# Dynamic convolution and MLP on one core: spreads of the weights' bounds in bf16, and the first scale of w_in ahead of the lo of x

## The chip, the cores and the metric

The kernel runs on one core of one Trainium2 chip. The metric is device microseconds of one launch, the median of several runs. Engines are named as in the profile: PE is TensorE's matmuls and PEld its weight loads, DVE is VectorE, ACT is ScalarE, POOL is GpSimd, SP issues most of the DMAs.

## The reference

Softmax weights over 7 taps and 8 heads make a causal dynamic convolution of x (4 x 4096 positions, 192 channels), and its result goes through a two-layer MLP with a leaky ReLU. All is float32.

```python
w = weight_gen - np.max(weight_gen, axis=-1, keepdims=True)
w = np.exp(w)
w = w / (np.sum(w, axis=-1, keepdims=True) + 1e-09)
x_pad = np.concatenate([np.zeros((B, pad, D), dtype=np.float32), x], axis=1)
idx = np.arange(S)[:, None] + np.arange(K)[None, :]
x_unf = x_pad[:, idx, :].reshape(B, S, K, H, group)
out = np.einsum('bshk,bskhg->bshg', w, x_unf).reshape(B * S, D)
h = out @ w_in                      # 16384 x 192 @ 192 x 2048
g = np.maximum(0.01 * h, h)
return (g @ w_out).astype(np.float32)   # 2048 x 192
```

## The kernel before

Each of the 128 partitions holds 128 consecutive positions, and a tile is 4 positions of each partition, so 512 rows; there are 32 tiles. The engines are programmed by hand, one function each (`pool`, `sp`, `act`, `dve`, `pe`), with semaphores between them; nothing reorders an engine's list.

The float32 products of the MLP are made from fp16 pieces. A value is scaled by a power of two, its fp16 rounding is the "hi", the remainder in fp16 the "lo"; a product is hi·hi + lo·hi + hi·lo (and some lo·hi of the last rows). The weights are split once at the start, in pieces of 512 columns: w_in into `whA`/`wlA` (its first 128 rows) and `whD`/`wlD` (its last 64 rows, with lo rows), w_out into `wo`. Each tile's x (the convolution's result) is split into `xs`, hi by ACT (`hi_of_x`), lo by DVE (`lo_of_x`, two instructions for each of the 4 rows of a tile), and transposed into `xT`: by TensorE for tiles 0 and 1, by DMA from tile 2 on.

A group of hidden units is 4 blocks of 128; there are 4 groups to a tile, and group n of the whole run is `hidden...(n)` on PE into the 4 banks `h_ps`. ACT makes `gh` (fp16) and `g` (float32) of each block in `leaky`, DVE or POOL subtracts them into `gl`, and PE projects `gh` and `gl` with `wo` into the output banks. A block of the next group may enter an `h_ps` bank when ACT's `g` of the former one is done (`s_g`).

The power of two for the weights comes from a bound, the sum of absolute values over rows. ACT sums |w_in| into `w_sum[:, 0, 0:3]` in three instructions (`abs_w_in`, semaphore `s_w_abs`) and |w_out| into `w_sum[:, 1, 0:3]` (`abs_wo`, `s_wo_abs`). `spread_top(n)` on PE (line 1248) brings the 128 partitions' sums to all partitions: three products of a column of `w_sum`, broadcast to 128 columns, with the identity `ident`, into `out_ps`. DVE's `w_scales(n)` then takes the maximum (line 843) and makes the scale of it in three small instructions (lines 655, 659, 664). n is 0 for w_in and 1 for w_out.

The order in the opening is this. PE: 15 junk products, `sum0` (the first tile's convolution added up by identity products in float32, line 1237), `spread_top(0)`, the transposes of tile 0's hi (line 994), 4 junk products, `hidden_by_pe(0)` (hi products at line 1022, transposes of the rest, lines 1027 to 1036 and 1105, 1108), `spread_top(1)`, then `first_steps` with `hidden_early(1)` (line 1049) and the projections (lines 1131, 1141). DVE: the softmax of the first taps, the products of the first convolution, `scales0`, row 0 of `lo_of_x(0)`, `w_scales(0)`, the hi piece of w_in that PE needs first (`split_hi(("A", 0))`, line 730), rows 1 to 3 of `lo_of_x(0)` (lines 743, 745), then `first_tile` with the lo pieces (line 735), `out_scale0` (with `w_scales(1)`), and `group(0)` (line 883). ACT: sums of |x|, of |w_in|, `hi_of_x(0)`, sums of |w_out| between copies of the transposed rows, then `leaky`.

Of the kernel before, what the change touches and what calls it, by code (L numbers as in the profile page):

```python
# [9 lines left out]
BF16 = mybir.dt.bfloat16  # L10
# [3 lines left out]
P = 128  # L14
# [51 lines left out]
def dynconv_mlp(nc, x, weight_gen, w_in, w_out, out):  # L66
    B, S, D = x.shape
    _, _, H, K = weight_gen.shape
    FF = w_in.shape[1]
    G = D // H  # L70
# [4 lines left out]
    SUB = 4  # L75
# [13 lines left out]
    with ExitStack() as ctx:  # L89
        def sb(name, shape, dt=F32):  # L90
            return ctx.enter_context(nc.sbuf_tensor(name, shape, dt))
# [15 lines left out]
        ident = sb("ident", [P, P])  # L107
# [4 lines left out]
        w_sum = sb("w_sum", [P, 2, 4])  # L112
# [173 lines left out]
        def sum0_of(j):  # L286
            return sums0[j // 2][:, j % 2 * D:(j % 2 + 1) * D]
# [324 lines left out]
        def _(dve):  # L612
# [26 lines left out]
            def softmax0(half, n):  # L639

                if n == 2:
                    dve.wait_ge(s_exp0, half + 1)
                elif n > 0:
                    dve.wait_ge(s_softmax0[half], n)
                r = slice(half * SUB * H, (half + 1) * SUB * H)
                softmax_op(half_taps(half).rearrange("p (r k) -> p r k", k=K), tap_stat[:, 0, r], tap_stat[:, 1, r], n
                           ).then_inc(s_softmax0[half], 1)
# [77 lines left out]
            def split_hi(piece):  # L725
                raw, hi, _ = pieces[piece]
                if piece[0] == "D":
                    dve.wait_ge(s_rawD[1 + (piece[1] > 0)], DMA)
                dve.wait_ge(s_w_scale, scales_done(piece))
                nc.vector.tensor_scalar(hi, raw, scale_of(piece), None, ALU.mult).then_inc(s_w_hi_v, 1)  # L730
# [3 lines left out]
                wait_hi(dve, piece)  # L734
                nc.vector.scalar_tensor_tensor(lo, raw, scale_of(piece), hi, ALU.mult, ALU.subtract).then_inc(s_w_lo, 1)

            def lo_of_x(t, first=0, last=SUB):

                for j in range(first, last):
                    x_j = sum0_of(j) if t == 0 else conv[:, j, :]  # L740

                    dve.wait_ge(s_x_hi, j // 2 * 2 + 2 if t == 0 else SUB * t + j + 1)
                    nc.vector.scalar_tensor_tensor(xs[:, j, 2 * P:3 * P], x_j[:, 0:P], x_scale[:, j:j + 1],  # L743
                                                   xs[:, j, 0:P], ALU.mult, ALU.subtract).then_inc(s_x_lo, 1)
                    nc.vector.scalar_tensor_tensor(xs[:, j, D:2 * P], x_j[:, P:D], x_scale[:, j:j + 1],  # L745
                                                   xs[:, j, P:D], ALU.mult, ALU.subtract).then_inc(s_x_lo, 1)
# [33 lines left out]
            def next_rows(m):  # L780

                convolve(m + 1, N_CONV - 1)
                lo_of_x(m + 1)
# [57 lines left out]
            def w_scales(n):  # L841
                dve.wait_ge(s_w_spread, n + 1)
                nc.vector.tensor_reduce(w_all[:, n:n + 1], out_ps[:, 1, 2 * n * P:2 * (n + 1) * P], AX_X, ALU.max).then_inc(s_w_back, 1)
                dve.wait_ge(s_w_back, n + 1)
                exponent(w_all[:, n:n + 1]).then_inc(s_w_scale, 1)
                dve.wait_ge(s_w_scale, 3 * n + 1)
                unscale_of(w_unscale[:, n:n + 1], w_all[:, n:n + 1]).then_inc(s_w_scale, 1)
                dve.wait_ge(s_w_scale, 3 * n + 2)
                scale_of_unscale(w_scale[:, n:n + 1], w_unscale[:, n:n + 1]).then_inc(s_w_scale, 1)
# [45 lines left out]
            def first_tile():  # L895
# [25 lines left out]
                group(2, 2, GROUP)  # L921
                lo_pieces(11, 12)
                lo_of_x(1)
                take_transposed(1)
                dve.wait_ge(s_chunk[1], DMA * 2)
# [42 lines left out]
            scales0()  # L968
            for n in range(2, 4):
                softmax0(1, n)  # L970
            lo_of_x(0, 0, 1)
            w_scales(0)
            split_hi(("A", 0))
            lo_of_x(0, 1, SUB)
            first_tile()
            second_tile()
            third_tile()
# [13 lines left out]
        def _(pe):  # L991
# [240 lines left out]
            def sum0():  # L1232
                for k in range(K - 1):

                    pe.wait_ge(s_prod0, 1 if k == 0 else k + 2 if k < K - 2 else K + 2)
                    for half in range(2):
# [3 lines left out]
                        if k == K - 2:  # L1240
                            ins.then_inc(s_sum0, 1)

            def spread_top(n):

                parts = ((0, 0), (1, 1), (2, 1))
                for k, (col, to) in enumerate(parts):
                    pe.wait_ge(s_w_abs if n == 0 else s_wo_abs, col + 1)
                    ins = nc.tensor.matmul(out_ps[:, 1, (2 * n + to) * P:(2 * n + to + 1) * P],
                                           w_sum[:, n, col:col + 1].to_broadcast([P, P]), ident[:], start=k == 0,
                                           stop=k == len(parts) - 1, skip_group_check=True)  # L1250
                ins.then_inc(s_w_spread, 1)

# [2 lines left out]
            pe.wait_ge(s_ident, 3)  # L1255
            sum0()
            spread_top(0)
            transpose_hi(0)
            warm_up(WARM_UP[1])
            hidden_by_pe(0)  # L1260
            spread_top(1)
            first_steps()
            for n in range(BY_PE * NG, N_GROUPS):
# [24 lines left out]
```

## Time and profile before

| what | us |
|---|---|
| median of 3 runs | 1034.67 |
| the runs | 1031.80, 1034.67, 1035.04 |
| the profiled execution | 1031.82 |
| its span, first to last instruction | 1030.0 |
| PE busy | 1021.7 (99%) |
| DVE busy | 938.8 (91%) |
| ACT busy | 634.3 (62%) |
| POOL busy | 550.8 (53%) |

The profile is of one execution, 28966 instructions long. Of its 40 equal slices PE has 39 at nine tenths or more, and the granted clock of TensorE is nine tenths or more in all. A busy PE is a modelled figure: matmuls are pipelined, so the starts are to be read rather than the durations. The opening, in which the weights are split, ends at about 50 us; the loop over tiles 2 to 31 follows.

### The profile page before, as it was taken

The numbers are of one execution on the slowest core, as the hardware profiler recorded it, in microseconds if no ns is written. First come the engines' busy times: TensorE is split into PE (matmuls) and PEld (weight loads), VectorE is DVE, ScalarE is ACT, GpSimd is POOL, SyncE is SP. The second block draws the span as 40 slices with busy tenths as digits, with TensorE's granted clock in tenths as the row PEclk, the third lists the DMA queues.
The fourth block names the chain that finished last, engine by engine and source line by source line (L and its number), as shares of the span: only waits on it lengthen the run. The fifth ranks groups of instructions, "written<-read, shape, count | busy, mean of one in ns | idle before, by whom it ended". The sixth has DMA issues, their size and how long they took to land.

```text
span 1030.0 us, 28966 instructions
## 1 busy us (share of the span) xinstructions
PE 1021.7 (99%) x12751; PEld 614.2 (60%) x12751; DVE 938.8 (91%) x1199; ACT 634.3 (62%) x1352; POOL 550.8 (53%) x375
## 2 busy tenths in 40 slices
PE   9999999999999999999999999999999999999998
PEld 4666655556556556655655655655565565566566
DVE  7989999999999999999999999999999999998611
ACT  7866665665556656556656555665565665566564
POOL 0114665555556655655655665565665566556543
PEclk9999999999999999999999999999999999999999
DMA  9421203112031310213112021210413112111100
GB/s 268 109 62 32 98 19 98 35 42 88 4 97 35 97 35 22 77 34 98 36 37 77 19 97 35 88 41 4 98 35 97 35 31 69 34 35 36 34 17 17
DMA packets 68309, 59.84 MB, mean 58 GB/s; under 512 B 56348, under 2 KB 60700, under 8 KB 66200
## 3 DMA queue, kind: packets, MB, share of 16 engines
q1 hardware_dynamic: 67196, 55.35, 18.2%
q0 software_dynamic: 864, 2.36, 1.3%
q8 instruction: 100, 1.64, 0.7%
q10 hardware_dynamic: 124, 0.29, 0.1%
q14 instruction: 25, 0.20, 0.1%
HBM read 29.34 MB, written 12.58 MB: 41 GB/s over the span
## 4 chain that ended last, share of the span: by engine, by line
PE 91%; DVE 6%; DMA 1%; ACT 1%; issue 0%; SPq 0%; POOL 0%; DVEq 0%; ACTq 0%; POOLq 0%
PE h_ps L1067 43%; PE out_ps L1177 22%; PE t_ps L1177 22%; PE out_ps L1131 1%; DVE prod L681 1%; PE h_ps L1049 1%; DVE gl L883 1%; DVE conv L697 1%; DMA rawD<-in_moe_w_in_dram 1%; PE out_ps L1141 1%; DMA prod<-prod 0%; DVE xs L743 0%; DVE xs L745 0%; ACT w_abs L559 0%; DVE gl L755 0%
## 5 line engine op out<-in xcount | busy, mean ns | idle before, releaser
L349 POOL TENSOR_TENSOR gl<-g,gh 128x512 f16<-128x512 f32 x360 | 543.5, 1536 | 411.1 <-ACT g L483 411.1
L481 ACT ACTIVATE gh<-h_ps 128x512 f16<-128x512 f32 x512 | 319.0, 623 | 370.8 <-PE h_ps L1067 361.0
L1177 PE MATMUL t_ps<-wo,gh 64*128 64x384 f16 (+1 forms) x1984 | 386.6, 317 | 0.9 <-ACT gh L481 0.9
L1177 PE MATMUL out_ps<-wo,gh 64*128 64x384 f16 (+1 forms) x1984 | 386.6, 317 | 0.0
L1067 PE MATMUL h_ps<-xT,whA 64*128 64x512 f16 x1920 | 364.3, 376 | 0.0
L483 ACT ACTIVATE g<-h_ps 128x512 f32<-128x512 f32 x512 | 323.4, 632 | 0.0
L681 DVE TENSOR_TENSOR prod<-xbuf,taps 128x768 f32<-128x768 f32 x186 | 273.3, 1485 | 0.0
L697 DVE TENSOR_TENSOR conv<-conv,prod 128x768 f32<-128x768 f32 x174 | 266.5, 1532 | 1.0
L1177 PE MATMUL t_ps<-wo,gl 64*128 64x192 f16 x1920 | 233.2, 243 | 1.4 <-DVE gl L755 1.4
L1177 PE MATMUL out_ps<-wo,gl 64*128 64x192 f16 x1920 | 233.2, 243 | 0.0
L1177 PEld LDWEIGHTS t_ps<-wo,gh 64*128 64x128 f16 x1984 | 181.3, 94 | 57.6 <-ACT gh L481 1.4
L1177 PEld LDWEIGHTS out_ps<-wo,gh 64*128 64x128 f16 x1984 | 181.3, 94 | 33.5
L1177 PEld LDWEIGHTS t_ps<-wo,gl 64*128 64x128 f16 x1920 | 169.0, 94 | 30.8 <-DVE gl L755 1.8
L1177 PEld LDWEIGHTS out_ps<-wo,gl 64*128 64x128 f16 x1920 | 169.0, 94 | 29.6
L1067 PE MATMUL h_ps<-xT,whD 64*128 64x512 f16 x960 | 182.2, 376 | 0.0
L1067 PE MATMUL h_ps<-xT,wlA 64*128 64x512 f16 x960 | 182.1, 376 | 0.0
L755 DVE TENSOR_TENSOR gl<-g,gh 128x512 f16<-128x512 f32 x120 | 108.6, 905 | 64.5 <-ACT g L483 62.9
L1067 PEld LDWEIGHTS h_ps<-xT,whA 64*128 64x128 f16 x1920 | 93.6, 94 | 99.7 <-issue 0.3
L1067 PE MATMUL h_ps<-xT,wlD 64*128 64x512 f16 x240 | 90.2, 376 | 0.0
L1067 PE MATMUL h_ps<-xT_again,wlD 64*128 64x512 f16 x240 | 90.2, 376 | 0.0
L1067 PEld LDWEIGHTS h_ps<-xT,whD 64*128 64x128 f16 x960 | 46.8, 94 | 56.8
L1067 PEld LDWEIGHTS h_ps<-xT,wlA 64*128 64x128 f16 x960 | 46.8, 94 | 42.6
(117 smaller groups left out, 715.0 us busy)
## 6 DMA issues: line engine op xcount, KB each, us to landing
xbuf<-in_x_dram SPq DMA_DIRECT2D x15, 1344.0 KB, 6.0
out_dram<-stage SPq DMA_DIRECT2D x31, 384.0 KB, 2.3
taps<-in_weight_gen_dram SPq DMA_DIRECT2D x16, 224.0 KB, 6.0
xT_again<-xT SPq DMA_DIRECT2D x29, 64.0 KB, 2.1
rawO<-in_moe_w_out_dram SPq DMA_DIRECT2D x4, 384.0 KB, 10.4
prod<-prod POOLq DMA_DIRECT2D x4, 384.0 KB, 4.3
rawA<-in_moe_w_in_dram SPq DMA_DIRECT2D x2, 512.0 KB, 8.0
xbuf<-in_x_dram SPq DMA_DIRECT2D x2, 384.0 KB, 7.0
```

What stands on the lines that cost most here:

```text
L349: nc.gpsimd.tensor_tensor(gl[:, q % RING, :], g[:, q % RING, :], gh[:, q % RING, :], ALU.subtract).then_inc(s_gl_p, 1)
L481: nc.scalar.activation(gh[:, q % RING, :], h_ps[q % GROUP][:], ACT.Prelu, alpha=SLOPE, scale=SHRINK0 if n < 2 * NG else SHRINK).then_inc(s ...
L483: nc.scalar.activation(g[:, q % RING, :], h_ps[q % GROUP][:], ACT.Prelu, alpha=SLOPE, scale=SHRINK0 if n < 2 * NG else SHRINK).then_inc(s_ ...
L681: ins = nc.vector.tensor_tensor(dst.rearrange("p (r g) -> p r g", g=G), rows, w.to_broadcast([P, SUB * H, G]), ALU.mult)
L697: ins = nc.vector.tensor_tensor(acc, acc, prod[:, k % PRODS, :], ALU.add)
L755: nc.vector.tensor_tensor(gl[:, q % RING, :], g[:, q % RING, :], gh[:, q % RING, :], ALU.subtract).then_inc(s_gl_v, 1)
L883: nc.vector.tensor_tensor(gl[:, at, :], g[:, at, :], gh[:, at, :], ALU.subtract).then_inc(s_gl_v, last - first)
L1049: nc.tensor.matmul(dst, w[:, c], xT_block(m % 2, b), start=w is whA and b == 0, stop=False)
L1067: ins = nc.tensor.matmul(h_ps[f % GROUP][:], w[rows, c], moved, start=first and half == f % 2, stop=last)
L1131: nc.tensor.matmul(out_of(m, j), gh[:, (m * NF + f) % RING, j * P:(j + 1) * P], wo[:, f, part, :], start=f == 0 and j % 2 == 0 and part == ...
L1141: ins = nc.tensor.matmul(out_of(m, j), gl[:, (m * NF + f) % RING, j * P:(j + 1) * P], wo[:, f, 0, :], start=False, stop=f == NF - 1, skip_ ...
L1177: ins = nc.tensor.matmul(dst, a[rows, (m * NF + f) % RING, j * P:(j + 1) * P], moved, start=i == 0 and k < 2 and a is gh and f == 0 and pa ...
```

## The change

Two things are changed. In `spread_top` both operands, a column of `w_sum` and the identity, are float32 tiles; now each is viewed as bf16 and every second element is taken, the upper 16 bits of each float32 (a cut without rounding; of 0 and 1 exact). The products are then bf16 products. Both spreads go through the function. On DVE, row 0 of `lo_of_x(0)` no longer stands ahead of `w_scales(0)` and the first hi piece, and the four rows follow in one call.

```diff
@@ DVE
-            def lo_of_x(t, first=0, last=SUB):
+            def lo_of_x(t):
-                for j in range(first, last):
+                for j in range(SUB):
@@ DVE, opening
             for n in range(2, 4):
                 softmax0(1, n)
-            lo_of_x(0, 0, 1)
             w_scales(0)
             split_hi(("A", 0))
-            lo_of_x(0, 1, SUB)
+            lo_of_x(0)
             first_tile()
@@ PE
+            def upper(a):
+
+                return a.bitcast(BF16).rearrange("p (n half) -> p n half", half=2)[:, :, 1]
+
             def spread_top(n):
@@
-                                           w_sum[:, n, col:col + 1].to_broadcast([P, P]), ident[:], start=k == 0,
+                                           upper(w_sum[:, n, :])[:, col:col + 1].to_broadcast([P, P]),
+                                           upper(ident[:]), start=k == 0,
                                            stop=k == len(parts) - 1, skip_group_check=True)
```

On DVE, behind the softmax of the second half of the first taps, before (xs is the split x, w_all the maximum, whA the hi piece):

```order
L625 TENSOR_SCALAR tap_stat<-tap_stat 128x32 [waits s_softmax01]
L743 SCALAR_TENSOR_TENSOR xs<-out_ps,x_scale,xs 128x128 [waits s_x_hi]
L745 SCALAR_TENSOR_TENSOR xs<-out_ps,x_scale,xs 128x64
L843 TENSOR_REDUCE w_all<-out_ps 128x1 [waits s_w_spread]
L655 TENSOR_SCALAR w_all<-w_all 128x1 [waits s_w_back]
L659 TENSOR_SCALAR w_unscale<-w_all 128x1 [waits s_w_scale]
L664 TENSOR_SCALAR w_scale<-w_unscale 128x1 [waits s_w_scale]
L730 TENSOR_SCALAR whA<-rawA,w_scale 128x512 [waits s_w_scale]
L743 SCALAR_TENSOR_TENSOR xs<-out_ps,x_scale,xs 128x128 [waits s_x_hi]
L745 SCALAR_TENSOR_TENSOR xs<-out_ps,x_scale,xs 128x64
```

and after:

```order
L625 TENSOR_SCALAR tap_stat<-tap_stat 128x32 [waits s_softmax01]
L843 TENSOR_REDUCE w_all<-out_ps 128x1 [waits s_w_spread]
L655 TENSOR_SCALAR w_all<-w_all 128x1 [waits s_w_back]
L659 TENSOR_SCALAR w_unscale<-w_all 128x1 [waits s_w_scale]
L664 TENSOR_SCALAR w_scale<-w_unscale 128x1 [waits s_w_scale]
L730 TENSOR_SCALAR whA<-rawA,w_scale 128x512 [waits s_w_scale]
L743 SCALAR_TENSOR_TENSOR xs<-out_ps,x_scale,xs 128x128 [waits s_x_hi]
L745 SCALAR_TENSOR_TENSOR xs<-out_ps,x_scale,xs 128x64
L743 SCALAR_TENSOR_TENSOR xs<-out_ps,x_scale,xs 128x128 [waits s_x_hi]
L745 SCALAR_TENSOR_TENSOR xs<-out_ps,x_scale,xs 128x64
```

The pair of row 0 moved from ahead of the maximum to behind the hi piece; five instructions passed it.

On PE, from the end of the first convolution's sum to the hi products of tile 0, before (a row with x3 or x4 is that many alike):

```order
L1237 MATMUL t_ps<-prod,ident 128x384
L1248 MATMUL out_ps<-ident,w_sum 128x128 [waits s_w_abs] x3
L994 MATMUL t_ps<-ident,xs 128x128 [waits s_x_hi]
L994 MATMUL t_ps<-ident,xs 128x128 x3
L1230 MATMUL h_ps<-junk 128x512 x4
L1022 MATMUL h_ps<-xT,whA 128x512 [waits s_w_hi_v,s_xT_a]
```

and after:

```order
L1236 MATMUL t_ps<-prod,ident 128x384
L1251 MATMUL out_ps<-ident,w_sum 128x128 [waits s_w_abs] x3
L993 MATMUL t_ps<-ident,xs 128x128 [waits s_x_hi]
L993 MATMUL t_ps<-ident,xs 128x128 x3
L1229 MATMUL h_ps<-junk 128x512 x4
L1021 MATMUL h_ps<-xT,whA 128x512 [waits s_w_hi_v,s_xT_a]
```

Nothing moved on PE; only the type in which the three products read their operands is another, and line numbers shift (1248 is now 1251, the lines between 743 and 1248 are one lower).

## Rows read from the trace of the kernel before

**Rows 1.** Busy us (instructions) of PE, PEld, DVE, ACT, POOL by stretch; then clock, DMA.

```profile
32.00:39.50 7.50, 7.18 (x58) 4.42 (x56) 7.50 (x10) 7.41 (x19) 2.72 (x3) 1.00 0.65 119
39.50:49.60 10.10, 10.04 (x88) 6.92 (x88) 9.84 (x14) 7.63 (x21) 0.00 (x0) 1.00 0.50 146
...
500.00:1000.00 500.00, 500.00 (x6408) 296.54 (x6406) 455.91 (x570) 304.65 (x649) 288.83 (x192) 1.00 0.17 48
```

**Rows 2.** Chain of waits, 15 to 24.5 us: start, us, what.

```profile
15.25 0.63 ACT xs L468 x2
...
18.32 0.26 DVE xs L743
18.57 0.19 DVE xs L745
...
19.02 0.20 DVE xs L745
```

**Rows 3.** Timeline of PE: start, us, group, [idle before <-releaser].

```profile
15.18 0.83 PE L1248 MATMUL out_ps<-ident,w_sum 128*128 128x128 f32 x6
16.55 0.40 PE L994 MATMUL t_ps<-ident,xs 128*128 128x128 f16 x4 [0.54 <-ACT xs L468]
...
18.01 1.02 PE L1022 MATMUL h_ps<-xT,whA 128*128 128x512 f16 x4 [0.21 <-DVE whA L730]
19.27 0.62 PE L994 MATMUL t_ps<-ident,xs 128*128 128x128 f16 x8 [0.24 <-DVE xs L745]
...
23.38 0.93 PE L1248 MATMUL out_ps<-ident,w_sum 128*128 128x128 f32 x6
24.15 0.38 PE L1049 MATMUL h_ps<-xT,whA 128*128 128x512 f16 x1
...
39.49 0.38 PE L1049 MATMUL h_ps<-xT,whA 128*128 128x512 f16 x1 [0.29 <-DVE wlD L735]
...
49.64 2.81 PE L1131 MATMUL out_ps<-wo,gh 128*128 128x192 f16 x32
```

**Rows 4.** Groups by line and shape, 13 to 25 us: busy us, mean ns, idle before.

```profile
L1248 PEld LDWEIGHTS out_ps<-ident,w_sum 128*128 128x128 f32 x12 | 1.6, 190 | 0.5 <-issue 0.2
...
L994 PE MATMUL t_ps<-ident,xs 128*128 128x128 f16 x12 | 1.0, 221 | 0.8 <-ACT xs L468 0.5 <-DVE xs L745 0.2
...
L994 PEld LDWEIGHTS t_ps<-ident,xs 128*128 128x128 f16 x12 | 0.7, 98 | 1.5 <-DVE xs L745 0.7 <-ACT xs L468 0.7
```

**Rows 5.** Timeline of ACT in the opening.

```profile
15.06 0.18 ACT L559 ACTIVATION_READ_ACCUMULATOR w_abs<-rawA 128x1 f32 x1
...
17.19 0.59 ACT L472 COPY xT<-t_ps 128x512 f16<-128x512 f16 x1
...
19.01 0.22 ACT L453 ACTIVATION_READ_ACCUMULATOR wo_abs<-rawO 128x1 f32 x1
...
25.74 0.65 ACT L483 ACTIVATE g<-h_ps 128x512 f32<-128x512 f32 x1
```

**Rows 6.** Timeline of DVE in the opening.

```profile
15.90 0.35 DVE L743 SCALAR_TENSOR_TENSOR xs<-out_ps,x_scale,xs 128x128 f16<-128x128 f32 x1 [1.00 <-ACT xs L468]
...
16.36 0.41 DVE L843 TENSOR_REDUCE w_all<-out_ps 128x1 f32<-128x256 f32 x1
...
17.38 0.49 DVE L730 TENSOR_SCALAR whA<-rawA,w_scale 128x512 f16<-128x512 f32 x1
...
24.35 0.42 DVE L843 TENSOR_REDUCE w_all<-out_ps 128x1 f32<-128x256 f32 x1 [0.42 <-PE out_ps L1248]
```

**Rows 7.** The loop: DVE's gl by line, one meeting with POOL, its stretch.

```profile
L755 DVE TENSOR_TENSOR gl<-g,gh x120: 677/680/1643, 93.5 to 1022.0; 128x512 f16<-128x512 f32 x120
...
229.18 4.70 POOL L349 TENSOR_TENSOR gl<-g,gh 128x512 f16<-128x512 f32 x3 [4.37 <-ACT g L483]
229.40 1.64 DVE L755 TENSOR_TENSOR gl<-g,gh 128x512 f16<-128x512 f32 x1
...
231.10 0.25 PE L1177 MATMUL t_ps<-wo,gl 64*128 64x192 f16 x1 [1.35 <-DVE gl L755]
...
220.00:250.00 30.00, 28.65 (x378) 17.28 (x376) 28.36 (x35) 16.77 (x35) 16.77 (x12) 1.00 0.26 84
```

**Rows 8.** Groups of PE, 1 to 7.3 us: the junk products at the start.

```profile
L1230 PE MATMUL h_ps<-junk 128*128 128x512 f16 x15 | 6.4, 616 | 1.2 <-DVE junk L948 1.2
```

## The prediction, made before the changed kernel ran

> **What bounds the kernel now.** I read the page first, then the busy time by stretch, then the engines' timelines of the opening, because all of the change lies before 25 us. TensorE has 99% of the span, and is busy for 500.00 of 500.00 us between 500 and 1000 us [rows 1]. So the time is the start of TensorE's dense work plus its length. The change takes nothing out of the loop over the tiles. It can only move the moment at which the loop is entered, and by no more than the slowest path to it moves.
>
> Two engines share the lead in the opening. Up to 24 us it passes between them: the chain goes from ScalarE's xs rows at 15.25 to VectorE, which holds it up to 19.22 (row 0 of lo of x, the scale of w_in, the first hi piece, rows 1 to 3), then to TensorE, and at 24.35 VectorE has waited 0.42 us for TensorE's second spread [rows 2, 6]. From there to 49.6 VectorE is nearly full (7.50 of 7.50 us, 9.84 of 10.10), and TensorE too [rows 1]. Where the two meet, TensorE starts right behind VectorE's pieces: hidden group 3 at 39.49 behind a wlD piece, and at 49.64 the products of the last w_out piece, whose lo VectorE makes just before [rows 3]. So what counts at the end is how much earlier VectorE's queue runs after its second maximum, with TensorE's own saving as the second bound.
>
> **The change, part by part.**
>
> *Spread 0 in bf16.* Before, three float32 products run as six matmuls from 15.18 to 15.18 + 0.83 = 16.01 [rows 3]. As bf16 there should be three like the transposes of x (128x128, 16 bits): a weight load of 98 ns and a product of 221 ns in the mean, and eight of them in 0.62 us, which with some 0.22 for the last leaves (0.62 - 0.22) / 7 = 0.057 us from start to start [rows 3, 4]. The third of them waits for ScalarE's last sum of |w_in|, there at 15.06 + 0.18 = 15.24 [rows 5]. With 0.04 us for a signal and 0.24 from load to end the spread is in PSUM at 15.52. VectorE, idle until 15.90 now, can start its maximum at about 15.60, one more signal and a rounding up. Bounds: not before 15.50 (the bare load and product), and not after 16.05 (as float32, and a signal). Plain 16-bit rows are the nearest to it, but none of them skips every second element, which is why I keep the float32 end.
>
> The Trainium skill, page "FP8 and Floating Point Precision", section "TensorE Precision Notes", has true float32 as four passes through the array; by it the products of a spread would shrink to a quarter, and the six matmuls for three products in the row agree with more than one pass. Its page "TensorE: Matmul & The Clock Gate", section "Back-to-back issue gap", speaks for less gain: about 81 ns a product of 128 columns in a stream of loads and products. By it three would take 0.24 us instead of the 0.17 used below, and the sum would stay, since VectorE is the later one there.
>
> *The scale and the first hi piece ahead of lo of x.* Before, VectorE idles 1.00 us for the xs rows, does row 0 at 15.90, and starts the maximum at 16.36 [rows 6]. After, the maximum starts at 15.60, **0.76 us** earlier. The scale follows, and the hi piece ends at 17.38 + 0.49 - 0.76 = 17.11 instead of 17.87. TensorE gets little from that directly: its hi products at 18.01 need also ScalarE's copy of the transposed rows, which ends at 17.19 + 0.59 = 17.78 and doesn't move [rows 3, 5]. That is 0.09 us, and hidden again, for the next thing on TensorE is the transposes at 19.27, and these wait for the last row of lo of x.
>
> Row 0 now stands behind the scale, and a row costs 0.26 + 0.19 = 0.45 us [rows 2]. The eight lo instructions end at 19.22 - 0.76 + 0.45 = 18.91: **0.31 us** earlier (bounds: 0.41 earlier, 0.14 later). TensorE's four hi products, started at 17.92, free it at 17.92 + 4 x 0.215 = 18.78, before that. From here all shifts by 0.31: the transposes to 18.96, the copies of them (ScalarE is free for them at 19.01 + 0.22 = 19.23), the lo piece of w_in, hidden group 0, and ScalarE's leaky activations [rows 3, 5].
>
> *Spread 1 in bf16.* Before, TensorE spends 23.38 to 24.15 on it, 0.77 us, and VectorE is ready at 24.35 - 0.42 = 23.93 [rows 3, 6]. After, three products occupy 3 x 0.057 = 0.17 us, so TensorE saves 0.60. The spread starts at 23.38 - 0.31 = 23.07 and is in PSUM by 23.07 + 0.11 + 0.24 = 23.42. VectorE's queue reaches it at 23.93 - 0.31 = 23.62, so VectorE itself is late now, and the maximum comes at 23.62: 24.35 - 23.62 = **0.73 us** earlier. Whether a product takes 0.06 or 0.11 us doesn't matter.
>
> *TensorE behind it.* It could enter hidden group 1 at 23.24 instead of 24.15, 0.91 us earlier. But the fourth block of the group needs the PSUM bank that ScalarE's fourth g frees; that g ends at 25.74 + 0.65 = 26.39 and moves by 0.31 only, to 26.08 [rows 5]. Each block is four products of 0.215 us, so the fourth starts at 24.15 + 3 x 0.86 = 26.73 before, and at 26.12 after: 0.61 us earlier. TensorE keeps that until it meets VectorE's pieces, which are 0.73 earlier. By 39.49, where it idled 0.29 us for wlD, it has 0.61 + 0.29 = 0.90 to spare and takes all of VectorE's 0.73 [rows 3]. The same at 49.64. What VectorE reads in between (ScalarE's hi pieces and g) was there earlier than it was asked for, since VectorE never idles; the DMA additions for tile 1 are started by its products and so move with it. Behind 49.64 TensorE is full, and the 0.73 stays.
>
> **Sum.** -0.76 + 0.45 = -0.31 at 19 us; a further -0.42, the idle time that goes at 24.35; together **-0.73 us**. Bounds: -0.83 (both spreads at their best) and +0.14 (bf16 no quicker, so that only the loss of the swap is left). The profiled execution took 1031.82 us with a span of 1030.0, so by it the sum is 1031.09. It lies at the low end of the runs of before (1031.80, 1034.67, 1035.04), which stand in two groups some 3 us apart. Against the median it is 1034.67 - 0.73 = 1033.94. A measurement here tells about 0.3%, 3.1 us, from no change, so the whole gain is under it.
>
> **The rivals.**
>
> *The same sum, but the median falls in the lower group.* Two of four executions of before lie near 1031.8. How such groups can come about: VectorE's gl takes 680 ns in the median and up to 1643 where GpSimd works on gl at the same time, and TensorE stalled 1.35 us behind one such here [rows 7]; a few more or fewer make 3 us. (The Trainium skill, "GPSIMD Engine Reference", section "1. Specifications", says that GpSimd shares its SBUF interfaces with VectorE instructions of two SBUF inputs; the trace agrees, 1643 against 677 ns.) Time: 1031.80 - 0.73 = 1031.07, 0.35% under the median of before.
>
> *Nothing gained, or a part.* If upper halves are read no faster than float32, all is 0.14 later: 1034.8. If ScalarE's 0.31 decides somewhere behind 24 us: 1034.4. For it: ScalarE is nearly full between 32 and 39.5 (7.41 of 7.50); against it: it has 2.47 us to spare up to 49.6 [rows 1].
>
> *Slower: the loop meets GpSimd in another phase.* Place: the 120 gl of VectorE in the loop. Price: 1.35 us where TensorE waits [rows 7]. One more such stall turns -0.73 into +0.6; three more make 1034.67 - 0.73 + 4.05 = 1037.99, 0.32% slower, and from there on it decides. For it: VectorE has little slack in the loop (455.91 of 500.00 us). Against: all engines shift together before 50 us, so their phase should be kept.
>
> *Slower: TensorE's clock falls in the opening.* Its idle time ahead of the hi transposes grows from 0.54 us to about 1.0 [rows 3]. Against: the granted clock reads 1.00 (2.4 GHz) in each stretch, also where TensorE idled 1.35 of 30 us [rows 1, 7]. For: the first junk products took 616 ns each, 6.4 / 15 = 0.43 us apart, where four hi products later take 1.02 us in all [rows 3, 8]. Some twenty products of 512 columns up to 24 us at 0.21 us more are 4.2 us: 1034.67 - 0.73 + 4.2 = 1038.1.
>
> **How the numbers follow.** The sum with the median in the upper group 0.60 (1033.9); the sum in the lower group 0.20 (1031.1, the one case faster by over 0.3%); nothing or a part 0.12 (1034.4 to 1034.8); the phase 0.05; the clock 0.03. So faster 0.20, same 0.72, slower 0.08. The predicted time is 1033.9. The range goes down to the lower group with the better bound and the 0.4 us by which runs of a group differ, 1031.80 - 0.83 - 0.4 = 1030.6, and up to the highest run with the loss of the swap and one more stall, 1035.04 + 0.14 + 1.35 = 1036.5.
>
> **What would show it.** Six matmuls of the spreads instead of twelve; the first maximum at about 15.6, the last lo row of x done at about 18.9, the second maximum at about 23.6 with VectorE no longer idle before it; hidden group 3 at about 38.8 and the products of the last w_out piece at about 48.9. If the second maximum still waits for TensorE, the bf16 product is slower than I take it. If the opening moves by 0.7 us and the time by more than 3, the loop is to be searched for stalls behind gl.

## The result, and the profile after

| | before | after |
|---|---|---|
| median of 15 runs | 1035.04 us | 1031.41 us |
| all runs | 1031.57 to 1036.40 | 1030.94 to 1032.92 |
| runs over 1034.3 us | 9 of 15 | 0 of 15 |
| median of the runs under 1034.3 us | 1031.80 | 1031.41 |
| profiled execution, its span | 1031.82, 1030.0 | 1031.87, 1030.1 |

The ratio of after to before is 0.9976, with a 95% interval of 0.9965 to 0.9987: some 0.24% less time. The interval leaves 1 out, but the difference is under the 0.3% that I said a measurement can tell. The two medians alone differ by 3.63 us, five times the sum of the prediction. The table shows where that comes from. Before has two groups of runs, 1031.57 to 1032.19 and 1034.67 to 1036.40, and after has the lower one only. Within the lower group the difference is 0.39 us by the medians and 0.63 by the lowest runs (1031.57 and 1030.94); but after also spreads wider, and four of its runs (1032.31 to 1032.92) lie above the highest of that group of before.

Both profiled executions fell into the lower group, so they can't show what is gone. They differ in the opening. PE of after, as in [rows 3]; the columns are start, us, group and idle time before it:

```profile
15.54 0.33 PE L1251 MATMUL out_ps<-ident,w_sum 128*128 128x128 bf16 x3
16.65 0.40 PE L993 MATMUL t_ps<-ident,xs 128*128 128x128 f16 x4 [0.78 <-ACT xs L468]
...
23.39 0.37 PE L1251 MATMUL out_ps<-ident,w_sum 128*128 128x128 bf16 x3
24.59 0.38 PE L1048 MATMUL h_ps<-xT,whA 128*128 128x512 f16 x1 [0.83 <-ACT g L483]
...
39.64 0.38 PE L1048 MATMUL h_ps<-xT,whA 128*128 128x512 f16 x1
```

A spread is three bf16 products in 0.33 to 0.37 us where six float32 ones took 0.83 and 0.93. But what the second one wins is lost at once: TensorE idles 0.83 us for ScalarE's first g, and hidden group 3 starts at 39.64 against 39.49 [rows 3]. ScalarE of after:

```profile
20.33 0.58 ACT L475 COPY xT_again<-t_ps 64x512 f16<-64x512 f16 x1
21.90 1.48 ACT L453 ACTIVATE wo_abs<-rawO 128x1536 bf16<-128x1536 f32 x1 [0.99 <-issue]
...
23.38 0.58 ACT L481 ACTIVATE gh<-h_ps 128x512 f16<-128x512 f32 x1
```

ScalarE idles 0.99 us ahead of the last sum of |w_out|, and the first leaky activation, next in its queue, starts at 23.38 (22.40 before). In the kernel this instruction waits for the third and fourth piece of w_out, and the chain of waits puts their DMA ahead of it:

```profile
10.57 10.33 DMA rawO<-in_moe_w_out_dram
20.90 0.99 issue
21.90 1.58 ACT wo_abs L453 x2
```

The 0.99 us called issue are a wait too. By the trace's semaphore records the last of the 16 shares of the fourth piece landed at 21.82, 0.08 us ahead of the instruction; in the kernel before it landed at 20.41, 0.51 us ahead. In six of the 14 profiles of this study the instruction starts at 21.70 to 22.99, each time 0.07 or 0.08 us behind that landing; in the others at 20.59 to 21.18. VectorE of after shows both sides, the win at the two maxima (0.45 and 0.50 us) and the wait for g that takes it back:

```profile
15.91 0.42 DVE L843 TENSOR_REDUCE w_all<-out_ps 128x1 f32<-128x256 f32 x1 [0.62 <-PE out_ps L1251]
...
23.85 0.42 DVE L843 TENSOR_REDUCE w_all<-out_ps 128x1 f32<-128x256 f32 x1
...
27.47 2.29 DVE L883 TENSOR_TENSOR gl<-g,gh 128x2048 f16<-128x2048 f32 x1 [0.45 <-ACT g L483]
```

So two questions were open: is the sum of 0.73 us right where w_out is in time, and what took the upper group away? For the second I had theory A (the groups come from the loop, and the change only shifts them) and theory B (something in the opening makes them, and the change removes it).

### The profile page after: what moved, and what is told of

It reads as the page before. It is cut to its first block, busy times and chain, and to the rows that moved or that the text cites. A ratio compares the mean times of both kernels' runs of the same rounds, so it can differ in the third digit from the quotient of the medians.

```text
span 1030.1 us, 28954 instructions
## 1 busy us (share of the span) xinstructions
PE 1020.6 (99%) x12745; PEld 612.6 (59%) x12745; DVE 939.0 (91%) x1199; ACT 634.3 (62%) x1352; POOL 550.5 (53%) x375
## 4 chain that ended last, share of the span: by engine, by line
PE 90%; DVE 6%; DMA 1%; ACT 1%; SPq 1%; issue 0%; POOL 0%; DVEq 0%; POOLq 0%
PE h_ps L1066 43%; PE out_ps L1176 22%; PE t_ps L1176 22%; PE out_ps L1130 1%; DVE prod L681 1%; PE h_ps L1048 1%; DMA rawO<-in_moe_w_out_dram 1%; DVE gl L883 1%; DVE conv L697 1%; PE out_ps L1140 1%; DMA prod<-prod 0%; DVE gl L755 0%; ACT g L483 0%; SPq L380 0%; ACT gh L481 0%
```

## Experiments: which part takes the upper group away

Four kernels on one chip, 12 runs each, beside 35 runs of the kernel before (20 of them over 1034.3, median 1035.35, median of the rest 1032.30).

**The kernel before, unchanged.** No edit.

> The kernel before, unchanged, beside itself: a second set of its times and a second profile. The 15 runs of before fall into 1031.6 to 1032.2 (6) and 1034.7 to 1036.4 (9), those of the changed kernel all lie in 1030.9 to 1032.9. Theory A (the sum of 0.73 us is right, and the groups come from the loop, where VectorE and GpSimd meet): again about half of the runs in each group, and a profile in the upper group shows its 3 to 4 us as TensorE stalls behind gl between 60 and 1000 us. Theory B (the upper group is made in the opening, before 60 us, and the change takes away what makes it): again both groups, and a profile in the upper group has its 3 to 4 us before 60 us. Ratio 1.000 by both.

Measured: 8 of 12 over 1034.3, median 1035.58, ratio 1.0005 (0.9988 to 1.0022). The groups are the kernel's own. Its profile is of the lower group.

**Only the bf16 spreads.**

```diff
-            w_scales(0)
-            split_hi(("A", 0))
-            lo_of_x(0)
+            lo_of_x(0, 0, 1)
+            w_scales(0)
+            split_hi(("A", 0))
+            lo_of_x(0, 1, SUB)
```

(against the changed kernel)

> Only the bf16 spreads, the order on VectorE as before. By my sum the first maximum stays at 16.4 (row 0 is ahead of it), the second moves from 24.35 to 23.93: 0.4 us. Theory A: both groups remain, each 0.4 us lower, median about 1034.6, ratio 0.9996. Theory B with the float32 products as the cause: the upper group is gone, median about 1031.5, ratio about 0.997.

Measured: 1 of 12 over 1034.3, median 1032.25, ratio 0.9989 (0.9975 to 1.0003). The second maximum starts at 23.74. With the bf16 spreads alone one run of 12 is left in the upper group, where before had 20 of 35.

**Only the order on VectorE.**

```diff
-            lo_of_x(0, 0, 1)
             w_scales(0)
             split_hi(("A", 0))
-            lo_of_x(0, 1, SUB)
+            lo_of_x(0)
```

(against the kernel before)

> Only the order on VectorE, the spreads in float32. By my sum the first maximum starts at 16.05 and lo of x ends 0.14 us later than before. Theory A: both groups remain, 0.1 us higher, median about 1035.1, ratio 1.0001. Theory B with the float32 products as the cause: the same as A. Theory B with the order on VectorE as the cause: the upper group is gone, median about 1032, ratio about 0.997.

Measured: 9 of 12 over 1034.3, median 1036.22, ratio 1.002 (1.0004 to 1.0036). The order does nothing for the groups. The three runs under 1034.3 have their median at 1033.19, 0.89 us above that of before where I had 0.14; what makes them so slow stays open. And this profile fell into the upper group, with a span of 1033.5, which let me look at it. Stretches of it (PE, PEld, DVE, ACT, POOL busy, then the granted clock as a share of 2.4 GHz):

```profile
188.00:192.00 4.00, 0.84 (x8) 0.20 (x4) 3.86 (x7) 3.99 (x9) 2.83 (x3) 1.00 0.01 2
192.00:194.00 2.00, 0.88 (x6) 0.50 (x8) 1.89 (x7) 1.39 (x5) 1.38 (x1) 0.74 0.00 0
194.00:196.00 2.00, 2.00 (x20) 1.36 (x18) 1.97 (x10) 0.00 (x0) 0.00 (x0) 0.50 0.49 197
196.00:198.00 2.00, 2.00 (x34) 1.53 (x32) 2.00 (x3) 0.00 (x0) 0.00 (x0) 0.91 0.54 125
```

and PE's row in it:

```profile
193.12 0.47 PE L1176 MATMUL t_ps<-wo,gh 64*128 64x384 f16 x1 [4.28 <-issue]
```

One stall of 4.28 us, and behind it the granted clock is 0.50 (1.2 GHz) between 194 and 196. The kernel before has two shorter stalls, 0.9 us for a gh at 189.5 and the 1.35 of [rows 7]; here these two are absent. By the three clock figures below 1.00 it ran at half speed for about 3.4 us, which costs half of that. As an estimate, 4.28 + 1.7 - 0.9 - 1.35 = 3.7 us is about the distance of the groups (the medians of the two groups of before are 1031.80 and 1035.78 in the first set). VectorE is late at that place:

```profile
189.24 1.57 DVE L620 TENSOR_TENSOR taps<-taps,tap_stat 128x448 f32<-128x448 f32 x1
190.73 1.64 DVE L755 TENSOR_TENSOR gl<-g,gh 128x512 f16<-128x512 f32 x1
192.29 0.40 DVE L777 SCALAR_TENSOR_TENSOR stage<-out_ps,out_scale,stage 128x192 f32<-128x192 f32 x1
```

against the kernel before, where the same three start 1.7 to 3.6 us earlier and the first two take less than half:

```profile
187.53 0.62 DVE L620 TENSOR_TENSOR taps<-taps,tap_stat 128x448 f32<-128x448 f32 x1
188.07 0.69 DVE L755 TENSOR_TENSOR gl<-g,gh 128x512 f16<-128x512 f32 x1
188.67 0.41 DVE L777 SCALAR_TENSOR_TENSOR stage<-out_ps,out_scale,stage 128x192 f32<-128x192 f32 x1
```

The stage rows empty the PSUM banks that TensorE's next projection needs: the second of them runs from 192.62 to 193.02, and TensorE goes on at 193.12. Following VectorE's list back, the lateness is gained in two steps. The second is at 110 us, where a product is due at the moment at which GpSimd takes up its gl. In the upper group's profile:

```profile
111.12 3.17 POOL L349 TENSOR_TENSOR gl<-g,gh 128x512 f16<-128x512 f32 x2 [3.71 <-ACT g L483]
111.35 1.91 DVE L681 TENSOR_TENSOR prod<-xbuf,taps 128x768 f32<-128x768 f32 x1
```

and in the kernel before:

```profile
110.81 0.95 DVE L681 TENSOR_TENSOR prod<-xbuf,taps 128x768 f32<-128x768 f32 x1
110.90 3.70 POOL L349 TENSOR_TENSOR gl<-g,gh 128x512 f16<-128x512 f32 x2 [4.04 <-ACT g L483]
```

VectorE's product starts 0.09 us ahead of GpSimd and takes 0.95 us, or 0.23 behind it and takes 1.91. The first step is at 71 us: VectorE waits for the last DMA addition of tile 2's products, 0.49 us in the kernel before, 0.30 in the changed one and 0.90 in the one of the upper group. The row of that wait, in the kernel before, in the changed one and in this one:

```profile
71.16 1.95 DVE L692 TENSOR_TENSOR conv<-conv,prod 128x768 f32<-128x768 f32 x2 [0.49 <-DMA prod<-prod]
```

```profile
71.00 1.95 DVE L692 TENSOR_TENSOR conv<-conv,prod 128x768 f32<-128x768 f32 x2 [0.30 <-DMA prod<-prod]
```

```profile
71.78 0.96 DVE L692 TENSOR_TENSOR conv<-conv,prod 128x768 f32<-128x768 f32 x1 [0.90 <-DMA prod<-prod]
```

**Both, with the second spread back in float32.**

```diff
-                                           upper(w_sum[:, n, :])[:, col:col + 1].to_broadcast([P, P]),
-                                           upper(ident[:]), start=k == 0,
+                                           (upper(w_sum[:, n, :]) if n == 0 else w_sum[:, n, :])[:, col:col + 1].to_broadcast([P, P]),
+                                           upper(ident[:]) if n == 0 else ident[:], start=k == 0,
```

> The changed kernel with the second spread back in float32. By my sum lo of x ends 0.31 us earlier and so does everything after it: 0.31 us. Theory A: both groups, median about 1034.7, ratio 0.9997. Theory B: if the first spread (or its order) is the cause the upper group is gone, median about 1031.9; if the second spread is the cause both groups remain.

Measured: none of 12 over 1034.3 (the highest are 1033.93 and 1034.05), median 1032.09, ratio 0.9984 (0.9969 to 0.9999).

**A new theory, F.** What can bf16 spreads at 15 and 23 us do to a DMA addition at 70 us? The packet records of the trace show a neighbour: instructions come in by DMA too, and queue 8 carries them in 100 packets of 16 KB. That these are PE's I take from how they move with the length of PE's list. A float32 product is two matmuls and two weight loads, a bf16 product one of each, so the change makes PE's list 12 instructions shorter (28966 and 28954 in all), and a fetch behind that place should fall 12 instructions later in the work. The stretch from 70.85 to 71.2 us, by DMA queue, in the kernel before:

```profile
q8 instruction: 1, 0.02, 17.3%
q0 software_dynamic: 1, 0.00, 0.2%
```

The addition (queue 0) has its last packet there, one of less than 512 bytes, and the 16 KB fetch starts at 70.87, as the last data packet ends. In the changed kernel this stretch has no packet, and the fetch comes at 71.87:

```profile
q8 instruction: 1, 0.02, 16.6%
```

From its first packet to its last the addition takes 68.49 to 70.65, 2.16 us, in the changed kernel, and no packet of it more than 0.28 us. In the kernel before it takes 68.46 to 70.88 with packets of 0.39 and 0.48 us; in the one of the upper group 68.67 to 71.31, with packets of 0.44, 0.48 and 0.42 us one after the other, and the fetch goes at 71.29, behind them. So theory F says: the fetch of PE's instructions meets the tail of the addition, VectorE gets it up to 0.6 us later, loses its lead of 0.09 us over GpSimd at 110 us, and TensorE stalls at 190. By it theory A has the place right, the loop, and theory B the origin, something in the opening. Rival G: the float32 products as such, or the time won in the opening, decide.

## Experiments: the fetch and the lateness

Four kernels on another chip, 12 runs each, beside 35 of the kernel before (13 over 1034.3, median of the others 1031.74).

**PE's 12 instructions put back** in the changed kernel: one junk product of 512 columns gives way to seven of 2 columns, each a product and a weight load.

```diff
             def warm_up(n):
                 for _ in range(n):
                     nc.tensor.matmul(h_ps[GROUP - 1][:], junk[:, 0:P], junk[:], start=True, stop=True)
+
+            def tiny(n):
+                for _ in range(n):
+                    nc.tensor.matmul(h_ps[GROUP - 1][:, 0:2], junk[:, 0:P], junk[:, 0:2], start=True, stop=True)
...
-            warm_up(WARM_UP[0])
+            warm_up(WARM_UP[0] - 1)
+            tiny(7)
```

> The changed kernel with PE's instruction count put back: one junk product of 512 columns in the first warm-up is replaced by seven of 2 columns, so PE's list is 12 instructions longer, as in the kernel before, at nearly the same time. The results of the first four runs: a profile with 1033.5 us of span shows PE idle for 4.3 us near 190 us and the clock at 0.50 behind it, VectorE 0.5 us late since its last wait for the DMA addition of tile 2 (at 71 us), and in that one the 16 KB fetch of PE's instructions lies on the tail of that addition; in the profiles without float32 spreads the fetch comes after it. Theory F (the fetch decides): the upper group comes back, half or more of the runs over 1034.5, median about 1035, ratio about 1.000; the profile's fetch near 70.9 us. Rival G (the float32 products or the time won in the opening decide, the count of instructions doesn't): no run over 1034.5, median about 1031.5, ratio 0.997.

Measured: 10 of 12 over 1034.3, median 1035.26, ratio 1.001 (0.9993 to 1.0027). The two others are 1030.97 and 1030.99. (One run is at 1034.35; by the bound of 1034.5 that I had named it is 9 of 12.) The upper group is back with 12 instructions that compute nothing, and bf16 products in the spreads. Rival G falls. In its profile, of the lower group, the fetch starts at 69.92 and the addition ends at 69.93, with packets of 0.36 and 0.48 us; VectorE waits 0.65 us and reaches the place at 110 us with 10 ns to spare:

```profile
110.04 0.95 DVE L681 TENSOR_TENSOR prod<-xbuf,taps 128x768 f32<-128x768 f32 x1
110.05 3.79 POOL L349 TENSOR_TENSOR gl<-g,gh 128x512 f16<-128x512 f32 x2 [3.95 <-ACT g L483]
```

**The kernel before with 8 PE instructions fewer**, all else as it was.

```diff
-            warm_up(WARM_UP[1])
```

> The kernel before without its four junk products ahead of hidden group 0, 8 PE instructions fewer, spreads in float32 and VectorE's order as before. Opening unchanged or 0.1 us earlier. Theory F: the fetch comes some 0.5 to 1 us later against the addition, and the upper group becomes rare: at most a quarter of the runs over 1034.5, median about 1032. Rival G: as the kernel before, more than half over 1034.5, median about 1035.3, ratio 1.000. If TensorE's clock needs these products, 2 us more in all runs.

Measured: none of 12 over 1034.3, median 1031.65, ratio 0.9986 (0.9973 to 0.9999); all runs lie within 1031.51 to 1031.94, where the lower group of before has its median at 1031.74. The fetch is at 71.19, the addition takes 2.16 us. This kernel has float32 spreads and the old order, and no upper group. The opening is the same to 0.01 us (the second maximum at 24.35), and the clock is 1.00 without those products.

**VectorE late by 0.43 us** in the changed kernel.

```diff
+        waste = sb("waste", [P, 448])
...
                 early_conv(2, ("sum", 1), ("out_scale", 0))
+                nc.vector.memset(waste[:], 0.0)
                 group(NG + 2)
```

> The changed kernel with a memset of 448 float32 on VectorE (about 0.5 us, nobody reads it) behind the convolution of tile 2, at about 74 us. If VectorE's lateness of half a us there is what makes the 4 us stall near 190 us (theories F and A agree on that), nearly every run lies over 1034.5: median about 1035, ratio about 1.000, and the profile shows the stall. If the lateness is only a companion of something else (rival G), the loop takes it up: median about 1031.5 to 1032.0, no stall of 4 us.

Measured: 12 of 12 over 1034.3 (11 over 1034.5), median 1035.53, ratio 1.0027 (1.0015 to 1.0039), although the fetch (70.49) is clear of the addition (67.72 to 69.88). The profile has the place at 110 us, now 0.04 us on the wrong side, and the stall with the half clock:

```profile
110.17 4.82 POOL L350 TENSOR_TENSOR gl<-g,gh 128x512 f16<-128x512 f32 x3 [3.90 <-ACT g L484]
110.21 1.92 DVE L682 TENSOR_TENSOR prod<-xbuf,taps 128x768 f32<-128x768 f32 x1
```

```profile
192.16 0.48 PE L1178 MATMUL t_ps<-wo,gh 64*128 64x384 f16 x1 [4.28 <-issue]
```

So lateness of VectorE is enough to make the stall, whatever made it late. The clock reads 0.50 for longer here, some 6.8 us from 190 us on by the same four stretches.

**Only the second spread in bf16**, 6 PE instructions fewer than before. The edit is that of the fourth kernel with `n == 1` for `n == 0`, and VectorE's order as before.

> Only the second spread in bf16: spread 0 in float32 and VectorE's order as in the kernel before, 6 PE instructions fewer. By my sum VectorE's second maximum is 0.42 us earlier. Theory F: the fetch moves by about 0.5 us against the addition, the upper group is rarer than before (between none and half of the runs), median 1031.8 to 1033. Rival G with the first float32 spread as the cause: as the kernel before but 0.4 us lower, more than half over 1034, median about 1034.8.

Measured: none of 12 over 1034.3, median 1031.17, ratio 0.998 (0.9966 to 0.9994), 0.57 us under the lower group of before (0.42 expected). The upper group goes without touching spread 0.

## Experiments: the sum, a candidate, and the point that decides

Four kernels on a third chip, beside 35 runs of before (15 over 1034.3, median of the others 1031.80).

**The changed kernel again.** No edit.

> The changed kernel unchanged, beside the kernel before on one chip. Theory F with my sum: no run over 1034.3; the lower group of before minus the median of these is the sum, 0.73 us (about 1031.8 against 1031.1). If the sum is worth less than I made it, the difference is 0.3 us or less.

Measured: none of 12 over 1034.3, median 1031.79, lowest 1030.98, ratio 0.9983 (0.9969 to 0.9997). Against the lower group of before that is 0.0 us by the medians and 0.53 by the lowest runs (1031.51). In its profile the last sum of |w_out| starts at 22.20, later than in any of before, and the span is 1030.4.

**The changed kernel without its second junk products**, the candidate.

```diff
-            warm_up(WARM_UP[1])
```

> The changed kernel without the four junk products ahead of hidden group 0. A candidate for a faster one. Theory F: the fetch comes later still, no run over 1034.3. The junk products end at 17.9 in the changed kernel, about when the hi products are ready anyway, so at most 0.1 us is won; if the clock needs them, TensorE runs at 1.2 GHz for a while in the opening and the median is 1 to 3 us higher.

Measured: none over 1034.3, median 1031.72, lowest 1030.97, ratio 0.9982 (0.9968 to 0.9997). No better than the changed kernel; the clock stays at 1.00.

**The order on VectorE and the second spread**, spread 0 in float32.

```diff
-                                           upper(w_sum[:, n, :])[:, col:col + 1].to_broadcast([P, P]),
-                                           upper(ident[:]), start=k == 0,
+                                           (upper(w_sum[:, n, :]) if n == 1 else w_sum[:, n, :])[:, col:col + 1].to_broadcast([P, P]),
+                                           upper(ident[:]) if n == 1 else ident[:], start=k == 0,
```

> The changed kernel with spread 0 in float32 again: the order on VectorE and spread 1 stay. By my sum the maximum starts at 16.1, lo of x ends 0.14 us later than before, VectorE's second maximum comes 0.42 - 0.14 = 0.28 us earlier than before, 0.45 later than in the changed kernel. Theory F: 6 PE instructions fewer than before, as with spread 1 alone, so no or hardly a run over 1034.3; median about 0.3 us under the lower group of before. If the upper group is there, it is the order on VectorE that brings it.

Measured: none over 1034.3, median 1031.54, all within 1031.45 to 1031.90, ratio 0.9979 (0.9966 to 0.9992). That is 0.25 us under the lower group of before, where I had 0.28 (0.3).

**VectorE late by a memset of 256.** The edit is that of the late kernel with 256 for 448.

> The changed kernel with a memset of 256 float32 on VectorE behind the convolution of tile 2, about 0.25 us, where 448 float32 (0.43 us) sent all 12 runs into the upper group. From the start of the first conv addition behind the wait to the next one took 1.24 to 1.45 us in profiles without the stall (1.60 in one) and 1.84 in the one with it. If VectorE's lateness decides at one point between 1.60 and 1.84, then 1.29 + 0.25 = 1.54 stays below: no run over 1034.3. If the upper group is already there in a good part of the runs, the point lies lower than the profiles say.

Measured: none over 1034.3, median 1031.36, ratio 0.9978 (0.9964 to 0.9992). But the reason I gave isn't the whole one: VectorE's product at 110 us is 0.09 us ahead of GpSimd again, as in the kernel before, so this lateness was taken up on the way. The traces show where. At 103 us VectorE has a small instruction that runs beside GpSimd's gl. In the changed kernel, before, this one, and that with 12 put back:

```profile
103.35 0.98 DVE L625 TENSOR_SCALAR tap_stat<-tap_stat 128x64 f32<-128x64 f32 x1
```

```profile
103.46 0.84 DVE L625 TENSOR_SCALAR tap_stat<-tap_stat 128x64 f32<-128x64 f32 x1
```

```profile
103.43 0.82 DVE L626 TENSOR_SCALAR tap_stat<-tap_stat 128x64 f32<-128x64 f32 x1
```

```profile
102.78 0.76 DVE L625 TENSOR_SCALAR tap_stat<-tap_stat 128x64 f32<-128x64 f32 x1
```

In all 14 profiles it ends 0.05 us behind the first of GpSimd's gl there, and the later it starts the less it takes, from 0.98 down to 0.76 us. So up to 0.22 us of lateness end at this instruction; only what is over goes on to 110 us. By profile, with the lateness counted at its start, from VectorE's addition at 70 us on and against the changed kernel:

| profile | PE instructions fewer | addition's packets over 0.3 us | fetch starts behind its end, us | wait at 71 us | late at 103 us | ahead of GpSimd at 110 us |
|---|---|---|---|---|---|---|
| before | 0 | 0.39, 0.48 | -0.01 | 0.49 | 0.15 | 0.09 |
| before again | 0 | 0.48 | 0.22 | 0.38 | 0.04 | 0.09 |
| 12 put back | 0 | 0.36, 0.48 | -0.01 | 0.65 | 0.32 | 0.01 |
| order alone, stall | 0 | 0.44, 0.48, 0.42 | -0.02 | 0.90 | 0.55 | -0.23 |
| three kernels | 6 | one, 0.44 to 0.48 | -0.01 to 0.19 | 0.38 | 0.03 to 0.05 | 0.08 to 0.10 |
| changed (two), bf16 alone, two without the second junk | 8, 12, 20 | none | 0.53 to 1.28 | 0.28 to 0.30 | 0.00 | 0.09 to 0.10 |
| memset of 256 | 12 | none | 0.58 | 0.29 | 0.17 | 0.09 |
| memset of 448, stall | 12 | none | 0.61 | 0.30 | 0.36 | -0.04 |

The lead at 110 us stays at 0.09 up to a lateness of 0.17, and falls by what is over 0.22, to within 0.02. The two profiles with the stall are the two in which VectorE comes behind GpSimd there.

Put together, all runs but those with the memset of 448, by the length of PE's list ahead of the loop (before is 0):

| PE instructions fewer | kernels | runs over 1034.3 us |
|---|---|---|
| 0 | before (five sets), order alone, 12 put back | 84 of 156 |
| 6 | three kernels | 0 of 36 |
| 8 | before without the second junk | 0 of 12 |
| 12 | changed (two sets), bf16 alone, memset of 256 | 1 of 51 |
| 20 | changed without the second junk | 0 of 12 |

The two tables fit: slow packets are there in all seven profiles with 0 or 6 instructions fewer and in none of the seven with 8 or more. With 6 fewer there was one in each, VectorE waits 0.38 us, and 0.04 late is taken up; with 0 fewer there were one to three, and the lateness goes up to 0.55.

What stays open. That the number of PE's instructions decides over the upper group is shown by runs, in both directions, and so is that lateness of VectorE makes the stall. That the fetch makes the addition's packets slow is argued from their coming together: it starts at their end or up to 0.22 us behind it, not beside them, and of the 0.35 us more that VectorE waits in the profile of the 12 put back only 0.16 lie in the addition's packets (2.32 against 2.16 us). Why one execution of the same kernel gets one slow packet and another three isn't known, and only one profile shows the upper group without a memset. A kernel that moves the fetch ahead of the addition wasn't tried.

## Why the prediction was right or wrong

**The range and the direction held** (1031.41 in 1030.6 to 1036.5), but it is the second case that came, the sum in the lower group, which had 0.20 (1031.1), and not the likeliest at 1033.9. That the number fell inside is no proof of the sum of 0.73 us: the range spans both groups, and most of the 3.63 us has a cause that the prediction didn't have. The measured ratio, 0.9976, is inside the 0.3% that I called the same; its interval, down to 0.9965, reaches over it.

**The step that failed** is "1034.67 - 0.73 = 1033.94" and the chance of 0.60 on it: I took the two groups as a chance that the change leaves alone. The runs show that it doesn't, none of 27 of the changed kernel against 65 of 132 of before. The first rival named the right pair, VectorE and GpSimd in the loop, but had the groups come from a few stalls of 1.35 us more or fewer; it is one stall of 4.28 us, decided by a product that meets GpSimd's gl at 110 us, and that rival too let luck choose the group. The sentence "all engines shift together before 50 us, so their phase should be kept" is where the argument broke. The engines do shift together. What doesn't is the fetch of PE's instructions, which goes by the count of instructions and not by time. I had counted the matmuls, twelve to six, as time on TensorE alone. The DMA queues stood in the page of the profile with "instruction" as a kind of its own, and I didn't ask when its packets fall.

**What the time hangs on** was right: the start of the dense work plus a fixed length. In the seven profiles without the stall in which w_out was in time (last landing at 20.16 to 20.90), of six kernels, before twice, the execution's time is the start of the second maximum plus 1007.46 to 1007.51 us.

**Spread 0 in bf16**: 0.33 us for three, which with 0.22 for the last is 0.055 from start to start (0.057 used). In the profile below it is in PSUM at 15.20 + 0.33 = 15.53; predicted 15.52. The bound from float32 wasn't needed: skipping every second element costs nothing that shows. This is the kernel with 12 instructions put back, in which w_out was in time:

```profile
15.57 0.42 DVE L843 TENSOR_REDUCE w_all<-out_ps 128x1 f32<-128x256 f32 x1 [0.62 <-PE out_ps L1255]
...
18.61 0.28 DVE L745 SCALAR_TENSOR_TENSOR xs<-t_ps,x_scale,xs 128x64 f16<-128x64 f32 x1
...
23.51 0.42 DVE L843 TENSOR_REDUCE w_all<-out_ps 128x1 f32<-128x256 f32 x1
...
48.79 2.40 PE L1130 MATMUL out_ps<-wo,gh 128*128 128x192 f16 x27
```

**The first maximum** is at 15.57 (predicted 15.60), the last row of lo of x ends at 18.89 (18.91), and the second maximum is at 23.51 (23.62), without idle time before it. **The products of the last w_out piece** start at 48.79 against 49.64 [rows 3], 0.85 us earlier (0.73), and hidden group 3 at 38.64 (about 38.8). Such closeness is in part luck. In this profile ScalarE's first xs row starts at 14.93, in that of before at 15.16, and in the second profile of the unchanged kernel at 14.89; there the second maximum is at 24.08 and not at 24.35. So it moved by 0.57 us against the one profile and by 0.84 against the other, and the 0.73 lies between. Some 0.1 us of the difference to my 23.62 comes in at the second maximum itself: I took the end of the instruction ahead of it as the time at which VectorE is ready, and without a wait it starts the next one some 0.08 us sooner. Two runs of that kernel are in the lower group, 1030.97 and 1030.99, 0.76 us under that of before. The order alone was to cost 0.14 us; its second maximum is at 24.58 against 24.35, but ScalarE's xs rows start 0.16 us later in that profile too. With the second spread in bf16 the order leaves 0.25 us, where that spread alone has 0.57 on another chip.

**The size of the gain in the mean** was too high, 0.39 and 0.0 us in the two comparisons of the changed kernel with the lower group. The term that was mis-sized is "all shifts by 0.31" at 19 us: for ScalarE it holds only if the last piece of w_out has landed in time. I never looked for that landing. It was at 20.41 in the profile of before and lies between 19.81 and 22.92 in the 14. Where it is late, it decides alone: in the five profiles without the stall in which it is at 21.66 or later, the execution's time is the landing plus 1010.02 to 1010.05 us, whatever the spreads and the order are, the changed kernel's two (21.82 and 22.12) among them. Set beside the constant of the second maximum, that makes an estimate of 23.62 - 2.56 = 21.06 for the latest landing with which my sum could hold. The rival nearest to it, "If ScalarE's 0.31 decides", shared a chance of 0.12. What sets the landing stays open: kernels that differ from the changed one by a few junk products had it at 20.16 and 20.38.

**The clock** didn't fall in the opening: the granted clock reads 1.00 there, also without the second junk products. That figure alone wouldn't do, since it reads 1.00 beside the first junk products at 0.43 us each too; but the four hi products behind an idle time of 0.90 us take 1.04 us in the changed kernel without those junk products, against 1.02 in before. It fell in the loop, at the stall of 4.28 us, which is part of the upper group's price and which I had not in any case.

## What to carry to other kernels

When the runs of a kernel form groups, find what makes them before adding a small gain to their median: here the groups were five times the gain, and a profile of the rare kind showed them in one row, a stall at a single place. An edit that adds or removes instructions can also move the fetches of that engine's program against all other DMAs; where a DMA's end is waited for, look at which packets lie on its tail. And look for the slack ahead of a meeting of two engines rather than at the lead in it: here the lead was 0.09 us in most profiles, but 0.22 us of lateness was taken up before it, and what went over that cost 4 us. Before a gain on one queue is added up, look up when each input lands that the other queues wait for.

## What the runs showed of the hardware that I had not expected

A 16 KB fetch of instructions near 70 us takes 0.88 to 1.41 us as one packet. In the seven profiles in which it starts at most 0.22 us behind the end of a 393 KB addition, one to three of the addition's last packets took 0.36 to 0.48 us; in the seven in which it starts 0.53 us or more behind, none took over 0.28. A bf16 matmul that reads the upper halves of float32 (every second element) ran as fast as one of dense 16-bit operands: three in 0.33 us, where four transposes of that shape take 0.40. VectorE's float32 product of 128x768 with two SBUF inputs takes 0.95 us if it starts 0.01 us ahead of GpSimd's instruction and 1.92 us if it starts 0.04 us behind it. A tensor_scalar of 128x64 beside GpSimd's gl took 0.76 to 0.98 us and ended 0.05 us behind the end of one of them in all 14 profiles; in the kernel before at 57.75, without GpSimd, it took 0.20. TensorE's granted clock was 0.50 for some 3.4 and 6.8 us in the two profiles with an idle time of 4.28 us, from about the end of that idle time on in the one and from 2 us ahead of it in the other, and 1.00 behind an idle time of 1.35.
